# Fused attention, soft mixture of experts and feed-forward layer: the first head's keys are loaded from ScalarE's queue, and its query pairs are added by VectorE

## Chip, core and metric

One core of a Trainium2 chip runs the whole program in one launch. The metric is the device time of one execution in microseconds (us). The kernel before took 743.18, 743.3 and 743.6 us in three timed runs; the median is 743.3.

## What is computed

Three stages follow each other. Attention has 32 heads (batch 4, 8 heads), 1152 keys of width 64, and queries that are averaged in pairs first, so 576 per head:

```python
q_pool = q.reshape(B, H, S // 2, 2, D).mean(axis=3)
scores = scale * np.matmul(q_pool, k.transpose(0, 1, 3, 2))
attn = np.exp(scores - np.max(scores, axis=-1, keepdims=True))
attn = attn / (np.sum(attn, axis=-1, keepdims=True) + 1e-09)
out = np.matmul(attn, v)
```

Then a soft mixture of experts (8 experts with 4 slots each: `logits = x @ phi`, softmax over the tokens into the slots, two weight matrices per expert, softmax over the slots back to the tokens), and last a layer `g(h) @ w_out` with `h = x @ w_in` (2304 tokens, 512 to 2048 to 512) and a piecewise g. All inputs and outputs are float32.

## The kernel before

The program is written out by hand for each engine: one block each for SyncE, GpSimd, TensorE, ScalarE and VectorE, each a list of instructions in fixed order. Engines meet only through semaphores (`wait_ge` on one side, `then_inc` on the other); a finished DMA adds 16.

Attention runs head by head. Per head, TensorE transposes keys and summed query pairs (`turn`, L576 to L598; `turn(m, 0)` holds the first eight key tiles at L585, `turn(m, 1)` the queries at L590 and the tail tiles at L594 and L596), multiplies for the row maxima (`row_max`, L600), turns the negated maxima (L634), multiplies scores (`scores`, L657 to L663), weighs the values (L680) and adds up the sums (L691). ScalarE rounds the transposed keys and queries to the high part (`high`, L1086; `round_k`, `round_q`) and takes the exponentials (L1072). VectorE computes the low part as a difference (`low`, L1328) and the row maxima (L1356). GpSimd adds the two queries of each pair (`prepare`, L469 to L476) and adds up exponentials. While head n is in its scores, head n+1 is in its maxima and head n+2 is being loaded.

Three buffers matter here. `k_raw` and `q_raw` take the keys and queries of one head as loaded, each by two DMAs: a large one (288 KB for keys, 256 KB for queries) and a small one of 32 KB. `q_pool` takes the added pairs. There is one of each, so head m's load waits until head m-1 has been read: a load of keys waits for `turned`, which counts two transposing jobs per head, and a load of queries for `q_pooled`. GpSimd's `prepare(m)` waits for `q_loaded` and, from head 1 on, for `turned`.

The start is a prologue of its own. SyncE issues `load_q(0)`, `load_k(0)`, `load_k(1)`, `load_q(1)` and `load_v(0)` (L371 to L375). GpSimd makes the identity `ident` (L464 to L466), waits for a small memset of VectorE (`mask_ready`) and prepares heads 0 and 1. TensorE transposes the identity 14 times into a bank that nothing reads (`warm(14, 0)`, L728), then does head 0's transposes. More such `warm` calls stand further down, between head 0's maxima (L733, L736, L744, L746). ScalarE starts with `round_k(0)` and `round_q(0)`, VectorE with memsets and small constants up to `consts_ready` (L1306 to L1325), then `low_k(0)` and `low_q(0)`, which wait for ScalarE. From L749 on the loop over the heads runs.

The end of the kernel has the only DMA that ScalarE issues (L1300): half of the last output tile, while SyncE issues the other half (L457).

Of the kernel before, what the change touches and what calls it, by code (L numbers as in the profile page):

```python
# [8 lines left out]
ALU = mybir.AluOpType  # L9
# [7 lines left out]
def soft_moe_chain(nc, q, k, v, phi, w1, w2, w_in, w_out, out):  # L17
# [13 lines left out]
    B, H, S, D = k.shape  # L31
# [3 lines left out]
    NT = S // P  # L35
    QT = 5
# [3 lines left out]
    PAIRS = H // 2  # L40
    TOK = B * SQ
    E, _, FE = w1.shape
    SLOTS = phi.shape[1]
    SPE = SLOTS // E
# [15 lines left out]
    def at(name, shape, offset, dt=F32):  # L60
        return nc.alloc_sbuf_tensor_at(name, shape, dt, offset=BASE + offset)


    QF = QT - 1
# [20 lines left out]
    k_raw = at("k_raw", [P, NT + 1, D], AFT)  # L85
    q_raw = at("q_raw", [P, QT, 2 * D], AFT + 2560)
    q_pool = at("q_pool", [P, QT + 1, D], AFT + 5120)
# [81 lines left out]
    with ExitStack() as ctx:  # L169
        ps = ctx.enter_context(nc.psum_tensor("ps", [P, 8, BANK], F32))  # L170

        def sem(name):
            return ctx.enter_context(nc.semaphore(name))

        ident_ready = sem("ident_ready")
        mask_ready, consts_ready = sem("mask_ready"), sem("consts_ready")
        k_loaded, q_loaded = sem("k_loaded"), sem("q_loaded")
        v_loaded = [sem(f"v_loaded{i}") for i in range(2)]
        q_pooled, rounded = sem("q_pooled"), sem("rounded")
        turned, turn_free = sem("turned"), sem("turn_free")  # L180
# [55 lines left out]
        k_dram = k.rearrange("b h (p j) d -> (b h) p j d", p=P)  # L236
# [99 lines left out]
        @block.sync  # L336
        def _(sp):
            def load_k(m):
                if m > 0:
                    sp.wait_ge(turned, 2 * m)  # L340
                sp.dma_start(k_raw[:, 0:NT, :], k_dram[m]).then_inc(k_loaded, 16)
                sp.dma_start(k_raw[:, NT, :], k_dram[m][:, NT - 1, :]).then_inc(k_loaded, 16)

            def load_q(m):
                if m > 0:
                    sp.wait_ge(q_pooled, m)
                sp.dma_start(q_raw[:, 0:QT - 1, :], q_big[m]).then_inc(q_loaded, 16)
                sp.dma_start(q_raw[0:QLAST, QT - 1, :], q_small[m]).then_inc(q_loaded, 16)
# [20 lines left out]
                                 inv_dram[:, HALF * h:HALF * h + HALF].to_broadcast([D, HALF])).then_inc(inverses_back, 16)  # L369

            load_q(0)  # L371
            load_k(0)
            load_k(1)
            load_q(1)
            load_v(0)  # L375
# [12 lines left out]
            for n in range(HEADS):  # L388
                if n + 2 < HEADS:
                    load_q(n + 2)  # L390
                    load_k(n + 2)
                if n + 1 < HEADS:
                    load_v(n + 1)
                if n == HEADS - 1:
                    sp.wait_ge(turned, 2 * HEADS)
                    sp.wait_ge(q_pooled, HEADS)
                    load_piece(PRE + STAGED)
                    sp.wait_ge(scores_ready, NT * (HEADS - 1))
                    for i in range(STAGED_EARLY):
                        load_piece(PRE + i)  # L400
                if n > 0:
                    turn_sums(n - 1)
                if 4 <= n < 4 + PRE:
                    load_piece(piece_first_in(n - 4))
# [58 lines left out]
        def _(pool):  # L463
# [5 lines left out]
            def prepare(m):  # L469

                pool.wait_ge(q_loaded, 32 * m + 32)
                if m > 0:
                    pool.wait_ge(turned, 2 * m)
                nc.gpsimd.tensor_tensor(q_pool[:, 0:QT, :], q_raw[:, :, 0:D], q_raw[:, :, D:2 * D], ALU.add)
                nc.gpsimd.tensor_tensor(q_pool[:, QT, :], q_raw[:, QF, 0:D], q_raw[:, QF, D:2 * D],
                                        ALU.add).then_inc(q_pooled, 1)  # L476
# [13 lines left out]
            def head(n):  # L490
                sums = (p_sum[:, :], p_sum2[:, :])
                if n > 1:
                    pool.wait_ge(q_pooled, min(n + 2, HEADS))
                    divide_x(n - 2)
                if n + 2 < HEADS:
                    prepare(n + 2)
                pool.wait_ge(exp_done, NT * n + 3)
                if n > 0:
                    pool.wait_ge(sums_done, n)
                    pool.wait_ge(probs_added, ADDS * n)  # L500
                nc.gpsimd.tensor_tensor(sums[0], probs[:, NT - 1, :], probs[:, 0, :], ALU.add).then_inc(probs_added, 1)  # L501
                pool.wait_ge(exp_done, NT * n + 5)
                nc.gpsimd.tensor_tensor(sums[1], probs[:, 1, :], probs[:, 2, :], ALU.add).then_inc(probs_added, 1)
                if n == HEADS - 1:
                    pool.wait_ge(probs_added, ADDS * n + 1)
                    nc.gpsimd.tensor_tensor(sums[0], sums[0], probs[:, 3, :], ALU.add).then_inc(probs_added, 1)
                else:
                    for u in (3, 4, 5):
                        pool.wait_ge(exp_done, NT * n + 5 + u // 4 * 2)
                        pool.wait_ge(probs_added, ADDS * n + u - 2)  # L510
                        total = sums[(u + 1) % 2]
                        nc.gpsimd.tensor_tensor(total, total, probs[:, u, :], ALU.add).then_inc(probs_added, 1)  # L512
                last = ADDS if n < HEADS - 1 else LAST_ADDS
                pool.wait_ge(probs_added, ADDS * n + last - 1)
                nc.gpsimd.tensor_tensor(sums[0], sums[0], sums[1], ALU.add).then_inc(probs_added, 1)

            pool.wait_ge(mask_ready, 1)
            prepare(0)
            pool.wait_ge(q_pooled, 1)
            nc.gpsimd.memset(q_neg[1][:, :].bitcast(F32), 0.0).then_inc(zeroed, 1)  # L520
            pool.wait_ge(zeroed, 1)
            prepare(1)
            for n in range(HEADS):
                head(n)
# [531 lines left out]
        def _(act):  # L1056
# [28 lines left out]
            def high(dst, src):  # L1085
                nc.scalar.activation(dst, src, ACT.Copy).then_inc(rounded, 1)  # L1086

            def round_k(m):
                act.wait_ge(turned, 2 * m + 1)
                high(k_hi[m % 2][:, 0:KP], ps[:, 6, :])  # L1090

            def round_q(m):
                kh, qh, b = k_hi[m % 2], q_hi[m % 2], tail_bank(m)
                act.wait_ge(turned, 2 * m + 2)
                for g in range(2):
                    for odd in range(2):
                        high(by_turns(qh, g, odd), turned_q(odd))
                high(kh[:, KP:KP + P], ps[:, b, 0:P])
                high(qh[:, P * QF:SQ], ps[:, b, P:P + QLAST])

            def place_neg_max(m):
# [4 lines left out]
                                                scale=neg_mask[0:r, t:t + 1])  # L1106
                last.then_inc(neg_free, 1)

            round_k(0)
            round_q(0)  # L1110
            round_k(1)
# [192 lines left out]
        def _(dve):  # L1304
# [18 lines left out]
                                  sum_ident[:, :].unsqueeze(1).to_broadcast([P, P // SLOTS, SLOTS]))  # L1323
            nc.vector.tensor_tensor(neg_mask[:, :], ident[:, 0:QT], ident[:, D:D + QT], ALU.add).then_inc(consts_ready, 1)
            dve.wait_ge(consts_ready, 1)  # L1325

            def low(dst, src, hi):
                return nc.vector.tensor_tensor(dst, src, hi.bitcast(F32), ALU.subtract)  # L1328
# [304 lines left out]
```

## Time and profile before

| | |
|---|---|
| timed runs, us | 743.18, 743.3, 743.6 |
| span of the profiled execution (first to last instruction), us | 738.7 |
| time of the profiled execution outside its span | not listed by itself; the timed runs lie 4.5 to 4.9 us above this span |
| TensorE busy | 724.9 us, 98% |
| VectorE, ScalarE, GpSimd busy | 71%, 62%, 66% |
| TensorE's share of the chain that ended last | 93% |
| mean granted TensorE clock | 0.995 of full |

The busy time is an average over all stages. The chain that ended last is followed back from the last instruction to what released it; a piece of it that gets shorter makes the kernel shorter until another wait ends later. In the names, PE is TensorE's matmuls, PEld its weight loads, DVE VectorE, ACT ScalarE, POOL GpSimd, SPq and ACTq the queues of SyncE and ScalarE where DMAs are issued. L12 is line 12 of the kernel.

### The profile page before, as it was taken

What the parts mean: (1) busy time and instruction counts of PE and PEld (TensorE: products, weight loads), DVE (VectorE), ACT (ScalarE), POOL (GpSimd) and SP (SyncE); (2) the same over time, 40 slices, a digit from 0 to 9 for tenths busy, and PEclk for the clock granted to TensorE, in tenths of its full rate; (3) what the DMA queues carried; (4) which work ended last, traced back from release to release, by engine and by line L of the source; (5) the groups of instructions that cost most, each with busy time, mean ns of one, the idle gap of its engine ahead of it and who ended that gap; (6) DMA issues with size and microseconds to landing.
All of it is one profiled execution on the core that took longest, in us unless ns stands there. A gap on an engine that the chain in (4) does not pass through costs nothing.

```text
span 738.7 us, 17096 instructions
## 1 busy us (share of the span) xinstructions
PE 724.9 (98%) x6375; PEld 540.5 (73%) x6375; DVE 523.4 (71%) x826; ACT 455.6 (62%) x1008; POOL 485.1 (66%) x431
## 2 busy tenths in 40 slices
PE   7999999999999999999999999999999999999997
PEld 5776777777777777777777677434778888888886
DVE  6888888888888888888888847533894555455542
ACT  3677776776777767767767763214655454545453
POOL 2588888888888888888888873212774444444442
PEclk8999999999999999999999999999999999999999
DMA  5123335334244353353342347899301010101011
GB/s 142 47 59 100 106 95 157 99 111 151 88 120 143 91 155 105 98 164 88 112 151 88 96 140 259 298 387 387 132 1 43 1 43 0 43 0 43 0 43 43
DMA packets 51623, 81.83 MB, mean 111 GB/s; under 512 B 14556, under 2 KB 20572, under 8 KB 51548
## 3 DMA queue, kind: packets, MB, share of 16 engines
q1 hardware_dynamic: 51468, 80.69, 35.0%
q8 instruction: 48, 0.79, 0.4%
q14 instruction: 27, 0.22, 0.1%
q10 hardware_dynamic: 80, 0.13, 0.0%
HBM read 75.94 MB, written 4.79 MB: 109 GB/s over the span
## 4 chain that ended last, share of the span: by engine, by line
PE 93%; DVE 3%; ACT 1%; issue 1%; POOL 1%; DMA 0%; SPq 0%; DVEq 0%; POOLq 0%; ACTq 0%
PE ps L680 20%; PE ps L657 8%; PE ps L987 8%; PE ps L986 8%; PE ps L985 8%; PE ps L625 6%; PE ps L659 5%; PE ps L661 5%; PE ps L663 5%; PE ps L691 3%; PE ps L585 3%; PE ps L975 2%; PE ps L899 2%; PE ps L869 2%; PE ps L590 1%
## 5 line engine op out<-in xcount | busy, mean ns | idle before, releaser
L1072 ACT ACTIVATE probs<-ps 128x576 f32<-128x576 f32 x288 | 183.8, 652 | 44.0 <-PE ps L663 28.9
L1356 DVE TENSOR_REDUCE mx<-ps 128x2 f32<-128x1024 f32 (+1 forms) x160 | 189.2, 1217 | 29.1 <-PE ps L625 27.1
L551 POOL TENSOR_TENSOR g_lo<-g_buf,g_hi 128x384 fp32r<-128x384 f32 x96 | 102.1, 1066 | 100.8 <-ACT g_hi L1245 100.8
L680 PE MATMUL ps<-probs,v_sb 128*64 128x288 f32 x1152 | 146.8, 409 | 0.1
L512 POOL TENSOR_TENSOR p_sum<-p_sum,probs 128x576 f32<-128x576 f32 x93 | 129.1, 1413 | 0.0
L1584 DVE SCALAR_TENSOR_TENSOR v_buf<-u_buf 128x384 f32<-128x384 f32 x96 | 60.2, 627 | 86.7 <-ACT u_buf L1238 86.1
L680 PEld LDWEIGHTS ps<-probs,v_sb 128*64 128x64 f32 x1152 | 79.7, 137 | 56.3 <-issue 5.2
L1238 ACT ACTIVATE u_buf<-ps,half 128x384 f32<-128x384 f32 x96 | 55.8, 582 | 93.7 <-PE ps L975 93.7
L985 PE MATMUL ps<-wo_hi,g_hi 128*128 128x512 f32 x282 | 110.5, 392 | 0.6 <-POOL g_lo L551 0.4
L987 PE MATMUL ps<-wo_lo,g_hi 128*128 128x512 f32 x282 | 110.8, 393 | 0.0
L986 PE MATMUL ps<-wo_hi,g_lo 128*128 128x512 f32 x282 | 110.6, 392 | 0.0
L657 PE MATMUL ps<-q_hi,k_hi 64*128 64x288 f32 x576 | 101.1, 335 | 0.7 <-ACT q_neg L1105 0.7
L659 PE MATMUL ps<-q_hi,k_lo 64*128 64x288 f32 x576 | 88.0, 292 | 0.0
L661 PE MATMUL ps<-q_lo,k_hi 64*128 64x288 f32 x576 | 87.9, 292 | 0.0
L663 PE MATMUL ps<-q_neg,k_one 64*128 64x288 f32 x576 | 87.3, 289 | 0.0
L501 POOL TENSOR_TENSOR p_sum<-probs 128x576 f32<-128x576 f32 x32 | 45.6, 1426 | 52.9 <-ACT probs L1072 52.9
L625 PE MATMUL ps<-k_hi,q_hi 64*128 64x512 f32 x320 | 70.6, 428 | 2.9 <-DVE mx L1356 1.6
L657 PEld LDWEIGHTS ps<-q_hi,k_hi 64*128 64x128 f32 x576 | 55.4, 184 | 23.8 <-ACT probs L1072 21.5
L985 PEld LDWEIGHTS ps<-wo_hi,g_hi 128*128 128x128 f32 x282 | 53.0, 188 | 14.3 <-issue 2.7
L1328 DVE TENSOR_TENSOR q_lo<-ps,q_hi 64x256 fp32r<-64x256 f32 (+1 forms) x160 | 60.5, 379 | 2.0 <-ACT q_hi L1086 0.7
L987 PEld LDWEIGHTS ps<-wo_lo,g_hi 128*128 128x128 f32 x282 | 52.9, 188 | 11.5
L659 PEld LDWEIGHTS ps<-q_hi,k_lo 64*128 64x128 f32 x576 | 57.3, 185 | 2.9
(214 smaller groups left out, 1251.6 us busy)
## 6 DMA issues: line engine op xcount, KB each, us to landing
pre<-in_moe_w SPq DMA_DIRECT2D x41, 512.0 KB, 4.7
k_raw<-in_k SPq DMA_DIRECT2D x32, 288.0 KB, 3.8
v_sb<-in_v SPq DMA_DIRECT2D x32, 288.0 KB, 2.8
q_raw<-in_q SPq DMA_DIRECT2D x32, 256.0 KB, 3.9
from_x<-in_moe_w SPq DMA_DIRECT2D x9, 512.0 KB, 5.2
p_inv<-inv_dram SPq DMA_DIRECT2D x62, 72.0 KB, 2.6
out<-o_stage SPq DMA_DIRECT2D x34, 128.0 KB, 2.4
staged<-in_moe_w SPq DMA_DIRECT2D x8, 512.0 KB, 5.2
```

The lines of the kernel that those rows point to most:

```text
L512: nc.gpsimd.tensor_tensor(total, total, probs[:, u, :], ALU.add).then_inc(probs_added, 1)
L625: mm = pe.matmul(ps[:, job_bank(m, j) + g, :], q_hi[m % 2][rows_of(g), P * t:P * t + P], k_hi[m % 2][rows_of(g), 0:KP], start=True, stop=True)
L657: mm = pe.matmul(out, k_hi[n % 2][rows, t], q_hi[n % 2][rows, cols], start=True, stop=False)
L659: mm = pe.matmul(out, k_lo[n % 2][rows, t], q_hi[n % 2][rows, cols], start=False, stop=False)
L661: mm = pe.matmul(out, k_hi[n % 2][rows, t], q_lo[n % 2][rows, cols], start=False, stop=False)
L663: mm = pe.matmul(out, k_one[rows, :], q_neg[n % 2][rows, cols], start=False, stop=True)
L680: mm = pe.matmul(ps[D * h:D * h + D, 4, 0:HALF], v_sb[n % 2][:, u, :], probs[:, u, HALF * h:HALF * h + HALF], start=(i == 0), stop=(i == N ...
L985: pe.matmul(o, g_hi[par][:, f, toks], wo_hi[:, f, :], start=(f == 0), stop=False)
L986: pe.matmul(o, g_lo[par][:, f, toks], wo_hi[:, f, :], start=False, stop=False)
L987: mm = pe.matmul(o, g_hi[par][:, f, toks], wo_lo[:, f, :], start=False, stop=(f == NF - 1))
L1072: nc.scalar.activation(dst, ps[:, b0:b0 + 2, 0:HALF], ACT.Exp, scale=SCORE_SCALE).then_inc(exp_done, 1)
L1356: top = nc.vector.tensor_reduce(mx[0:w, NC * t:NC * t + 2], ps[0:w, b:b + 2, :], AX.X, ALU.max)
```

## The change

The two DMAs that load head 0's keys are issued by ScalarE, as the first entries of its list after the helpers, and no longer by SyncE. Head 0's query pairs are added by VectorE, behind its constants, with the same two additions that GpSimd's `prepare(0)` made. GpSimd's wait for `mask_ready` goes; the memset that it waited for is on VectorE's own list ahead of the additions. `load_k` and `prepare` are now called for heads from 1 on only, and their waits lose the test for head 0.

```diff
         def _(sp):
             def load_k(m):
-                if m > 0:
-                    sp.wait_ge(turned, 2 * m)
+                sp.wait_ge(turned, 2 * m)
...
             load_q(0)
-            load_k(0)
             load_k(1)
...
             def prepare(m):
                 pool.wait_ge(q_loaded, 32 * m + 32)
-                if m > 0:
-                    pool.wait_ge(turned, 2 * m)
+                pool.wait_ge(turned, 2 * m)
...
-            pool.wait_ge(mask_ready, 1)
-            prepare(0)
             pool.wait_ge(q_pooled, 1)
             nc.gpsimd.memset(q_neg[1][:, :].bitcast(F32), 0.0).then_inc(zeroed, 1)
...
+            nc.scalar.dma_start(k_raw[:, 0:NT, :], k_dram[0]).then_inc(k_loaded, 16)
+            nc.scalar.dma_start(k_raw[:, NT, :], k_dram[0][:, NT - 1, :]).then_inc(k_loaded, 16)
             round_k(0)
             round_q(0)
...
             dve.wait_ge(consts_ready, 1)
+            dve.wait_ge(q_loaded, 32)
+            nc.vector.tensor_tensor(q_pool[:, 0:QT, :], q_raw[:, :, 0:D], q_raw[:, :, D:2 * D], ALU.add)
+            nc.vector.tensor_tensor(q_pool[:, QT, :], q_raw[:, QF, 0:D], q_raw[:, QF, D:2 * D],
+                                    ALU.add).then_inc(q_pooled, 1)
```

## Rows read from the trace of the kernel before

**Rows 1.** The page: busy time of each engine, and the chain that ended last by engine.

```profile
PE 724.9 (98%) x6375; PEld 540.5 (73%) x6375; DVE 523.4 (71%) x826; ACT 455.6 (62%) x1008; POOL 485.1 (66%) x431
...
PE 93%; DVE 3%; ACT 1%; issue 1%; POOL 1%; DMA 0%; SPq 0%; DVEq 0%; POOLq 0%; ACTq 0%
```

**Rows 2.** Chain of waits in order of time, 0 to 45 us: start, us, what.

```profile
2.44 2.94 DMA k_raw<-in_k
...
6.72 0.26 ACT q_hi L1086
...
19.63 0.40 PE ps L657 x2
...
28.61 4.52 PE ps L680 x36
```

**Rows 3.** Timeline, SyncE: start us, us, engine, line, operation, out<-in.

```profile
0.74 0.40 SPq L347 DMA_DIRECT2D q_raw<-in_q  x1
...
1.83 0.57 SPq L341 DMA_DIRECT2D k_raw<-in_k  x1
```

**Rows 4.** Timeline, TensorE's matmuls from 3.7 us; in brackets idle before, releaser.

```profile
3.72 1.06 PE L728 MATMUL ps<-ident 128*128 128x128 f32 x4
5.43 0.66 PE L585 MATMUL ps<-ident,k_raw 128*128 128x128 f32 x4 [0.65 <-DMA k_raw<-in_k]
```

**Rows 5.** Timeline, ScalarE, GpSimd and VectorE up to 7 us.

```profile
0.74 1.28 ACT L1086 ACT_TABLE_LOAD   x1 [0.74 <-PEq L1622]
...
3.77 0.86 POOL L474 TENSOR_TENSOR q_pool<-q_raw 128x320 f32<-128x320 f32 x1 [2.30 <-DMA q_raw<-in_q]
4.59 0.32 POOL L475 TENSOR_TENSOR q_pool<-q_raw 128x64 f32<-128x64 f32 x1
...
6.13 0.60 ACT L1086 ACTIVATE k_hi<-ps 128x512 fp32r<-128x512 f32 x1 [4.11 <-PE ps L585]
...
6.83 0.69 DVE L1328 TENSOR_TENSOR k_lo<-ps,k_hi 128x512 fp32r<-128x512 f32 x1 [3.75 <-ACT k_hi L1086]
```

**Rows 6.** Stretches: length, busy us by engine, granted clock, DMA share, GB/s.

```profile
1.75:2.75 1.00, 1.00 (x6) 1.00 (x6) 0.96 (x6) 0.27 (x1) 0.00 (x0) 1.00 0.86 236
2.75:3.75 1.00, 1.00 (x7) 1.00 (x6) 0.30 (x2) 0.00 (x0) 0.00 (x0) 1.00 0.74 131
3.75:4.75 1.00, 1.00 (x5) 0.63 (x3) 0.00 (x0) 0.00 (x0) 0.97 (x2) 1.00 0.71 244
4.75:5.40 0.65, 0.03 (x1) 0.00 (x0) 0.00 (x0) 0.00 (x0) 0.59 (x2) 1.00 0.07 19
```

**Rows 7.** DMA issues by line, 730 to 739 us: KB each, median us to landing.

```profile
out<-o_last SPq DMA_DIRECT2D x1, 128.0 KB, 2.3
out<-o_last ACTq DMA_DIRECT2D x1, 128.0 KB, 2.6
```

**Rows 8.** Lines L728 (1 to 5 us) and L585 (5 to 6.5): ns min/median/max.

```profile
L728 PE MATMUL ps<-ident x14: 421/421/477, 1.5 to 4.4; 128*128 128x128 f32 x14
...
L585 PE MATMUL ps<-ident,k_raw x4: 272/273/331, 5.4 to 5.8; 128*128 128x128 f32 x4
```

**Rows 9.** VectorE's additions and subtractions: L1388, and L1328 up to 20 us.

```profile
L1388 DVE TENSOR_TENSOR p_rest<-probs x1: 896/896/896, 443.9 to 443.9; 128x576 f32<-128x576 f32 x1
...
L1328 DVE TENSOR_TENSOR q_lo<-ps,q_hi 128x64 fp32r<-128x64 f32 x2 | 0.4, 215 | 0.0
```

**Rows 10.** Stretches around the low clock, columns as in rows 6.

```profile
12.00:12.10 0.10, 0.10 (x4) 0.10 (x1) 0.10 (x1) 0.00 (x0) 0.10 (x1) 0.77 0.08 10
12.10:18.80 6.70, 6.26 (x28) 4.22 (x25) 6.11 (x14) 3.32 (x11) 1.86 (x4) 0.50 0.60 167
18.80:18.90 0.10, 0.10 (x1) 0.00 (x0) 0.10 (x1) 0.10 (x2) 0.00 (x0) 0.60 1.02 343
```

**Rows 11.** Timeline, 15 to 18 us: two operations that waited.

```profile
15.12 0.69 DVE L1350 TENSOR_REDUCE mx<-ps 128x4 f32<-128x512 f32 x1 [0.53 <-PE ps L620]
...
17.41 0.48 PE L634 MATMUL ps<-ident,neg_max 128*128 128x128 f32 x1
```

## The prediction

> **What bounds the kernel now.** I read the page first: TensorE is busy for 98% of the 738.7 us span and is 93% of the chain that ended last [rows 1]. So a change pays only if it moves TensorE's work as a whole. The chain in order of time shows where that can happen: until about 20 us it jumps between a DMA, ScalarE, VectorE and TensorE, and from the first head's weighing at 28.61 us it is TensorE without a gap [rows 2]. The change touches only the first 7 us. An advance that survives to the first scores matmul at 19.63 us shifts all that follows by as much, because every later load, addition and exponential waits for a semaphore of this same stream of work and none for a point in time.
>
> The head of the chain is the first load of keys: SyncE issues it as its third and fourth DMA (1.83 and 2.44 us), it lands at 2.44 + 2.94 = 5.38, the transposes of L585 start at 5.43, ScalarE rounds the keys from 6.13 and the queries from 6.72 [rows 2 to 5]. TensorE's row before it says what is late next: its 14 transposes of the identity (L728) end at 4.78, and only 0.65 us idle stands before L585, released by the DMA [rows 4]. That 0.65 us, or little more, and not the 1.1 us by which the load can be issued earlier, is the size of the prize.
>
> **Part 1: the keys' two DMAs leave SyncE for ScalarE.** Removed from SyncE: two issues, the first of 0.57 us [rows 3]. Nothing there gets earlier by it: what follows there is the second head's keys, whose load waits until both transposing jobs of the first head have ended (`turned` at 2), with or without the change. Added on ScalarE: two issues ahead of everything it does. Its engine is free: one table load at 0.74 for 1.28 us, then idle for 4.11 us until 6.13 [rows 5]. Put first, they start at 0.74 and, with SyncE's durations for them, at 0.74 + 0.57 + 0.04 = 1.35, instead of 1.83 and 2.44: 1.09 us earlier. The table load then runs from about 1.8 to 3.1 and is hidden.
>
> Issued 1.09 us earlier, the keys land at 5.38 - 1.09 = 4.29 if nothing disturbs them. But now they run beside the queries, issued in the same microsecond. The DMA windows show the engines busy for 0.86 + 0.74 + 0.71 + 0.05 = 2.36 us of each engine's time between 1.75 and 5.4, with only 0.07 x 0.65 = 0.05 us of it behind 4.75, so the last bytes come near 4.85 and the semaphore at 5.38 [rows 6]. The same work at the fullest share shown for a microsecond (0.86) takes 2.74 us from 1.75, to 4.49, which is 0.36 earlier: landing at 5.02. Packed without a gap it takes 2.36, to 4.11: landing at 4.64. Bounds 4.29 and 5.38 (no gain at all); I take 4.75, nearer to the packed case, since two queues leave fewer gaps than one. The nearest row for two DMAs issued at one moment on the two queues is the end of the kernel: 128 KB each, 2.3 us to landing on SyncE's and 2.6 on ScalarE's [rows 7]; ScalarE's queue is no slower than some tenths.
>
> The Trainium skill bears on this: DMA: Bandwidth & Descriptors, section "Issuing engines are not separate DMA queues", says that DMAs started from different engines share the same 16 DMA engines and interleave, and that using several saves only the sequencer's time to issue them. By that rule the gain is at most the 1.09 us of issue, no time below 742.2 comes out, and the queries' bytes take their part of it; the trace before can't show it for loads, since all of them go through one queue.
>
> **What is late next.** TensorE's warm-up. Its last four matmuls take 1.06 us, the last alone 0.42, so they follow each other by (1.06 - 0.42) / 3 = 0.21; the last starts at 4.36 and ends at 4.78, and the next can start near 4.6 [rows 4, 8]. With the keys at 4.75 + 0.05 the first transposes start at 4.8, 0.63 us earlier.
>
> Part of this is paid back by the clock. The 14 warm transposes take 421 ns each, those of L585 272 [rows 8]: the first ran at the low level (1.2 GHz) although the granted clock reads 1.00 in their rows [rows 6], the second at the high one (2.4). The rise lies between 4.4 and 5.43. Transposes started at 4.8 meet it either way. If it is there already, nothing is lost; if it comes only at 5.43, the four take 3 x 0.21 + 0.42 = 1.05 us instead of 0.66, 0.4 lost. I take 0.15, since a rise in the middle of the 0.6 us leaves one or two slow ones. Gain at the rounding of the keys: 0.63 - 0.15 = 0.48, bounds 0.2 and 0.8 (the start at 4.6).
>
> **Part 2: the query pairs are added by VectorE.** Removed from GpSimd: 0.86 + 0.32, from 3.77 to 4.91 [rows 5]. Before, this was early: the keys' transposes began 0.5 us behind it. After part 1 it would nearly bind (4.91 against the queries' first transpose at 4.8 + 0.4), so moving it protects the gain rather than adds to it. VectorE's two additions are not in the trace; its row for 128x576 in SBUF takes 896 ns and that for 128x64 215 [rows 9], so 1.33 ns a column: 0.55 us for the 128x320 one and 0.2 for the 128x64 one, 0.75 together; bounds 384 x 1.33 = 0.5 (nothing fixed per instruction) and 1.18 (GpSimd's own). With the queries landing where they did (3.7) that ends at 4.5. Delayed by the keys to 4.75 it ends at 5.5; the four transposes of queries and ends then end some 0.7 later (four of L585 take 0.66 [rows 4]), 6.2, while ScalarE, rounding the keys for 0.6 from about 5.65, wants them at 6.25. Covered by 0.05; I count nothing, and 0.15 in the bad case. Behind the waiting addition on VectorE stands only the low part of the keys, which came at 6.83 after 3.75 us of idleness [rows 5] and now comes near 6.35. Its constants are done where that idleness begins, 6.83 - 3.75 = 3.08, before the queries land. GpSimd's memset of q_neg and second preparation follow the sum's semaphore and the second load, as before. The wait that load_k and prepare lose their `if` for is no new wait for any head above 0.
>
> **Sum.** 0.5 us off the first 20. Up to 19.63 the rest is work of engines released by each other, and part of it is TensorE at the low clock (granted 0.50; the shares 0.77 and 0.60 of the slices at its ends put it from 12.05 to 18.88 [rows 10]); all of it moves along. Span 738.7 - 0.5 = 738.2. The three timed runs lie 4.5 to 4.9 above the span; with the median's 4.6 that is 742.8 us. A difference under 0.2% (1.5 us) is what a measurement of this kernel can't tell from no change, so this is "same".
>
> **Rivals.**
> 1. The clock comes back later (slower). The granted clock falls at 12.05, when TensorE has just had idle stretches, and rises at 18.88, 0.75 before the first scores [rows 10]. The first scores now come at 19.1. For: the rise leads them by 0.2 only, if it keeps its time, and nothing ties it to the work. Against: the activity before it is the same, moved by half a microsecond. Price: time at the low level does half its work, so each us of it behind 19.1 loses 0.5 where TensorE bounds. The change turns slower than before once it lasts 1.0 us beyond, and slower by 0.2% from 4.0 us beyond. Half of the whole low stretch again (3.4 us) loses 1.7: 744.0.
> 2. The clock doesn't fall, or falls later. Then L620 no longer keeps VectorE idle for 0.53 us, and L634 takes 0.27, as a transpose at the high level, instead of 0.48 [rows 8, 11]: 0.7 us more, 742.1. For: less idleness before 5.4. Against: the idle pieces behind 7 us are unchanged.
> 3. ScalarE's table load goes first, so the change doesn't do what it says. The load's row bears the line of the first activation, but ran at 0.74, long before that was released [rows 5], so its place against the DMAs is open. Then they start at 2.06 and 2.67, 0.23 later than now: 743.5. It decides once the second issue starts behind 2.44. The Trainium skill, ScalarE: Activation LUTs, section "Step-by-step: what each stage is for", says that the compiler has placed the load right before the ACTIVATE that needs it; by that, the DMAs go first and the forecast stands. No row here decides it.
> 4. The transfers are hidden in each other: both sets land where the keys did, about 5.2 to 5.4, and the additions now end near 6.0. Then VectorE's sum is late for ScalarE by some tenths: 743.3, no gain. The shares of 0.6 to 0.9 in the windows speak against that much [rows 6].
>
> **How the numbers follow.** Forecast (gain 0.2 to 0.9): 0.6. Rival 1: 0.1, of which 0.04 beyond 744.8. Rival 2: 0.1, of which 0.04 below 741.8. Rival 3: 0.1. Rival 4: 0.1. So faster by over 0.2% 0.04, slower 0.04, same 0.92. The range takes rivals 2 to 4 and the cheap half of rival 1, and the 0.4 us by which the three runs differ: 741.9 to 743.7.
>
> **What would show it.** Two DMA issues on ScalarE at 0.74 and 1.35, the table load behind them; L585 starting near 4.8, perhaps with matmuls of 421 ns among its four; VectorE's sum of 0.75 us ending by 5.5; the first scores near 19.1; the same distance from there to the end. Wrong if L585 stays at 5.4, if ScalarE's first issue is at 2.06, if the clock's rise stands behind the first scores, or if the time leaves 741.8 to 744.8.

## The result, and the profile after

In 22 timed runs each, taken in turns on one chip, the kernel before has a median of 743.21 us (740.4 to 744.57) and the changed one 741.5 us (739.76 to 742.72): ratio 0.9981, 95% interval 0.9973 to 0.9989, so 0.8 to 2.0 us faster. Two more comparisons gave 0.9988 (0.9976 to 1.0) and 0.9984 (0.997 to 0.9997). The three together put the gain at 0.9 to 1.4 us; the second interval just reaches no gain. Forecast were 0.5 us and 742.8, with a range from 741.9; the time lies below it. All runs that count here are of one state; one single run of the kernel before, beside the later experiments, took 2024.64 us and is in no median or ratio.

Each run now comes with its span. Over 46 runs of the changed kernel the time is 1.8 us above the span, and it is 1.8 us for before too (the prediction used 4.6). So the profiled execution of before, with its span of 738.7, took about 740.5 us by that distance: it was as quick as the fastest of the 22 runs (740.4), and not one like the median. The changed kernel's profiled execution took 741.45 us with a span of 739.7. Set side by side, the two profiles show the change as 1.0 us slower. That is the first thing to know before comparing their lines.

The page of the changed kernel, busy time and chain that ended last (answers to [rows 1]):

```profile
PE 726.1 (98%) x6375; PEld 541.8 (73%) x6375; DVE 524.3 (71%) x828; ACT 455.1 (62%) x1008; POOL 483.7 (65%) x429
...
PE 94%; DVE 3%; issue 1%; POOL 1%; ACT 1%; POOLq 0%; DVEq 0%; ACTq 0%
```

Its timeline up to 7 us (answers to [rows 3 to 5]; L580 is L585 of before, L585 is L590, L1081 is L1086):

```profile
0.74 0.41 ACTq L1104 DMA_DIRECT2D k_raw<-in_k  x1
...
1.19 0.46 ACTq L1105 DMA_DIRECT2D k_raw<-in_k  x1
...
1.67 1.28 ACT L1081 ACT_TABLE_LOAD   x1 [1.67 <-PEq L1623]
...
4.57 1.11 PE L580 MATMUL ps<-ident,k_raw 128*128 128x128 f32 x4
4.76 0.49 DVE L1324 TENSOR_TENSOR q_pool<-q_raw 128x320 f32<-128x320 f32 x1 [1.68 <-DMA q_raw<-in_q]
5.17 0.22 DVE L1325 TENSOR_TENSOR q_pool<-q_raw 128x64 f32<-128x64 f32 x1
5.44 0.29 PEld L585 LDWEIGHTS ps<-ident,q_pool 128*128 128x128 f32 x2 [0.17 <-DVE q_pool L1325]
...
6.60 1.59 ACT L1081 ACTIVATE q_hi<-ps 64x256 fp32r<-64x256 f32 x4 [0.28 <-PE ps L591]
```

The keys are issued first and the table load runs behind them. The keys land at 1.19 + 3.3 = 4.5, and in this profile the warm-up (which ends at 4.78, as before) is what the transposes follow. The queries are no longer there at 3.77 but at 4.76, and VectorE's sum ends at 5.39, when TensorE has waited 0.17 us for it. ScalarE rounds the queries at 6.60, against 6.62 in the timeline of before (6.72 in its chain [rows 2]): next to nothing was won in this profile up to there, because the four transposes took 1.11 us and not 0.66 [rows 4] and those of the queries behind them were slow too.

The granted clock of the changed kernel (answers to [rows 10], columns as in rows 6):

```profile
16.00:17.00 1.00, 0.53 (x4) 0.29 (x3) 0.97 (x5) 0.00 (x0) 0.56 (x2) 0.92 0.86 299
17.00:23.00 6.00, 5.33 (x36) 4.82 (x37) 4.75 (x10) 2.68 (x7) 0.00 (x0) 0.50 0.26 77
23.00:24.00 1.00, 1.00 (x13) 0.93 (x11) 0.84 (x2) 0.65 (x1) 0.19 (x1) 0.66 0.00 0
...
474.00:480.00 6.00, 6.00 (x46) 1.71 (x42) 0.32 (x2) 0.00 (x0) 0.00 (x0) 0.72 1.05 403
```

The low stretch is as long as in the first profile, 6.8 us, but lies from 16.84 to 23.68 and so inside the first head's scores (which start at 18.95, not 19.63). A second one lies at the start of the experts' first product (0.72 on average from 474 to 480), which takes 15.4 us instead of 13.8. Rivals 1 and 2 of the prediction are about such stretches. They turn up in the profiles of both kernels below, so an experiment has to hold them still before the change can be measured. (The product's time here and below is from the start of its first matmul to that of its last.)

### The profile page after: what moved, and what is told of

Read it like the earlier page. It is cut to its first block, busy times and chain, and to the rows that moved or that the text cites. A ratio compares the mean times of both kernels' runs of the same rounds, so it can differ in the third digit from the quotient of the medians.

```text
span 739.7 us, 17095 instructions
## 1 busy us (share of the span) xinstructions
PE 726.1 (98%) x6375; PEld 541.8 (73%) x6375; DVE 524.3 (71%) x828; ACT 455.1 (62%) x1008; POOL 483.7 (65%) x429
## 4 chain that ended last, share of the span: by engine, by line
PE 94%; DVE 3%; issue 1%; POOL 1%; ACT 1%; POOLq 0%; DVEq 0%; ACTq 0%
PE ps L675 20%; PE ps L652 9%; PE ps L982 8%; PE ps L981 8%; PE ps L980 8%; PE ps L620 6%; PE ps L654 5%; PE ps L656 5%; PE ps L658 5%; PE ps L686 3%; PE ps L580 3%; PE ps L970 2%; PE ps L864 2%; PE ps L894 2%; PE ps L585 1%
## 5 line engine op out<-in xcount | busy, mean ns | idle before, releaser
L982 PEld LDWEIGHTS ps<-wo_lo,g_hi 128*128 128x128 f32 x282 | 53.0, 188 | 11.4
```

What stands on the lines that cost most here:

```text
L982: mm = pe.matmul(o, g_hi[par][:, f, toks], wo_lo[:, f, :], start=False, stop=(f == NF - 1))
```

## The experiments

Two theories follow from these profiles: **prologue** (the order of loads and sums is shorter by itself) and **clock** (the change moves low-clock stretches). Times are medians; ratios are to the kernel before on the same chip.

### The two kernels again

> The kernel before, unchanged, against itself. The profile that the prediction used had a span of 738.7 us at a mean granted clock of 0.995, while 22 runs have a median of 743.2; the changed kernel's runs lie 1.75 us above their spans. Clock theory: the spans of typical runs are near 741.4 us at a mean clock under 0.990, and the new profile shows more low-clock time in the first 30 us than the 6.8 us of the first one. Prologue theory (the time was won in the order of loads and sums, the clock is the same for both kernels): clocks like the changed kernel's, 0.988 to 0.995. Ratio 1.000 within 0.001 by both.

Measured: 742.55 us, ratio 0.9995 (0.9986 to 1.0004); mean clocks of single runs 0.988 to 0.999. Its profile is another one than that of [rows 2 to 5]. The chain of waits:

```profile
2.44 2.84 DMA k_raw<-in_k
...
5.33 1.11 PE ps L585 x4
6.44 0.43 PE ps L590 x2
...
7.33 0.38 ACT q_hi L1086
```

The keys land as before, but TensorE stays at its low level through all of their and the queries' transposes, and the queries are rounded at 7.33, 0.7 later. The low stretch goes from 14.1 to 24.3. Span 740.8, which is what the median less 1.8 gives; the first profile was 2 us below that. The clocks of single runs are not all under 0.990, as the clock theory had them.

> The kernel before again: ratio 1.000 within 0.001. The first weighing near 30 us, not the 28.5 of the first profile, if that one was a lucky case; the experts' product either 13.8 or 15.4.

Measured: 742.94, ratio 0.9997 (0.9981 to 1.0012). Queries rounded at 7.44, low from 12.5 to 26.1, first weighing at 31.3 (later than the expected 30), experts 15.4, span 742.4. Of three profiles of this kernel the first is the quickest, a lucky case.

> The changed kernel again, on one chip with the three below. In the first profile of before the queries landed at 3.7 us and the keys' transposes ran at the high clock; in a second profile of the same kernel they landed at 4.5 and the transposes took 1.11 instead of 0.66 us, so the first was a good case. Prologue theory: at equal granted clock the changed kernel is 0.3 to 0.6 us shorter, because late queries no longer meet GpSimd's 1.14 us sum and a late start of the keys; ratio 0.9992, time 0.6 below before. Clock theory: the spread of 4 us between runs is where the low-clock stretch falls, and more than 1 us of the 1.7 us is a better mix of it: ratio 0.998, and a mean clock of the runs clearly above that of before.

Measured: 741.89, ratio 0.9988 (0.9976 to 1.0). Queries rounded at 6.53, weighing at 29.2, experts 13.8, span 738.9. Its runs' clocks (mostly 0.988 and 0.993) are no better than before's: the mean over all 46 runs of the changed kernel is 0.991, over 136 of before 0.993. In every trace the record of the granted clock begins only where the level first rises. The low start ahead of it is read as 1.00, so the mean clock doesn't order the kernels: in the 136 runs of before, those at 0.998 have spans from 738.2 to 742.8.

> The changed kernel again. Own-gain theory with two clocks: 0.8 to 1.4 us below before, the first weighing near 29.2 us in the profile, the experts' product either 13.8 or 15.4.

Measured: 742.11, ratio 0.9984 (0.997 to 0.9997). Queries rounded at 6.38, weighing at 30.2 (the forecast of 29.2 missed: low from 11.4 to 25.1), experts 15.4.

### Each half alone

> Head 0's keys from ScalarE's queue, the pairs still added by GpSimd. Both theories: keys land near 4.5, queries near 4.7, GpSimd's sum of 1.14 us ends at 5.9, so ScalarE's rounding of the queries starts at 7.1, 0.5 later than in either kernel. Clock theory: the idle 0.65 us in front of the keys' transposes is gone, so most of the 1.7 us stays: 741.8 to 742.3. Prologue theory: 0.5 us slower than before, 743.7.

Measured: 741.87, ratio 0.9998 (0.9987 to 1.0009). Before took 742.18 beside it. Queries rounded at 7.52, later than expected; the time is inside the clock theory's range, but the ratio shows no gain and no loss: neither theory's size came. Its profile shows why a mean clock misleads: it reads 0.998, and yet TensorE's first rise comes only at 20.46 us. And the end of this kernel is 0.4 us shorter than before (see the table below), which hides part of what the late queries cost.

> Head 0's pairs added by VectorE, the keys still on SyncE's queue. Keys land at 5.38 as before, TensorE idles 0.65 us before their transposes, the sum ends near 4.5 and is not waited for. Clock theory: same as before, 743.2 (742.8 to 743.6). Prologue theory: also 743.2, since the sum was not late. A gain of more than 0.8 us would speak against both.

Measured: 742.57, ratio 1.0001 (0.9992 to 1.001), the same as before, as both theories had it.

> The kernel before with 17 instead of 14 identity transposes at the start, so that TensorE is busy until about 5.4, when the keys land; no load or sum is moved. Clock theory (what TensorE's idle 0.65 us at 4.8 did to the granted clock later is what the change removed): 741.5 to 742.2, mean clock like the changed kernel's. Prologue theory: 743.2, or 0.1 to 0.2 us more where the keys' transposes wait for the last of the 17.

```diff
-            warm(14, 0)
+            warm(17, 0)
```

Measured: 742.25, ratio 1.0002 (0.9993 to 1.0011). The clock theory in this form falls: filling the idle 0.65 us alone gives nothing by the ratio, with a low stretch from 11.5 to 25.2 all the same. The interval leaves room for 0.5 us, so a small gain of this edit isn't excluded.

### The keys hold up the queries

> The changed kernel with ScalarE issuing the keys' DMAs only when the queries have landed. If the keys' packets are what delays the queries (4.7 us in the changed kernel's profile), the queries land by 3.4 to 3.8 here and the keys 2.5 to 3 us later, 6.2 to 6.8, and TensorE idles for them. If the queries' landing varies by itself, it may be anywhere from 3.4 to 4.7. Time 1 us longer or more: 742.5 to 744.

```diff
+            act.wait_ge(q_loaded, 32)
             nc.scalar.dma_start(k_raw[:, 0:NT, :], k_dram[0]).then_inc(k_loaded, 16)
```

Measured once: 745.37 us, above the expected 742.5 to 744; a single run says little of the time. Its timeline does say something:

```profile
3.83 0.49 DVE L1325 TENSOR_TENSOR q_pool<-q_raw 128x320 f32<-128x320 f32 x1 [0.75 <-DMA q_raw<-in_q]
...
6.85 1.12 PE L580 MATMUL ps<-ident,k_raw 128*128 128x128 f32 x4 [2.08 <-DMA k_raw<-in_k]
```

Queries at 3.8 here; at 4.76 to 5.20 in all six profiles of the changed order and at 5.06 to 5.18 with the keys alone on ScalarE's queue; at 3.7 to 4.6 where SyncE issues all four. So keys that are issued beside the queries make these land later: the means over the profiles of the changed order and of those in which SyncE issues all four are 5.0 and 4.0, 1.0 us apart. The Trainium skill's page DMA: Bandwidth & Descriptors, section "Issuing engines are not separate DMA queues", says that DMAs started from different engines interleave on the same 16 DMA engines, and the traces of the changed order agree: in each of its six profiles both sets land within 0.3 us of each other.

### The clock held up

More identity transposes go where TensorE waits for ScalarE or VectorE, in both kernels ("more": the first three lines; "full": all).

```diff
             turn(0, 1)
-            warm(5, 0)
+            warm(12, 0)
             row_max(0, 0)
             row_max(0, 1)
-            warm(5, 0)
+            warm(12, 0)
...
-            warm(5, 5)
+            warm(8, 5)
...
             slot_sums_of_tails()
+            warm(7, 1)
             pe.wait_ge(fold_w_ready, 1)
...
+            warm(3, 1)
             pe.wait_ge(sim_ready, 1)
```

> The changed kernel with more identity transposes in TensorE's gaps of the prologue: 12, 12 and 8 in place of 5, 5 and 5. They fit into waits for VectorE or ScalarE at the high clock (0.11 us each). Clock theory: the low stretch between 11 and 25 us goes or gets shorter, the spread between runs shrinks, and the time is 1 to 2 us below the changed kernel's (739.8 to 740.5). Prologue theory alone: no gain, or up to 0.5 us slower where a transpose at the low level (0.21 us) delays the maxima.

Measured: 739.46, ratio 0.9961 (0.9947 to 0.9975), runs from 739.28 to 740.18. The stretches of its profile:

```profile
5.00:12.00 7.00, 5.83 (x40) 4.57 (x41) 4.90 (x9) 2.50 (x7) 1.24 (x2) 1.00 0.52 140
12.00:19.00 7.00, 4.66 (x34) 3.06 (x33) 6.92 (x15) 3.88 (x12) 1.68 (x4) 1.00 0.60 173
19.00:26.00 7.00, 6.73 (x79) 5.71 (x79) 6.39 (x9) 4.32 (x7) 2.73 (x2) 1.00 0.01 2
```

No low stretch is left up to 26 us; TensorE is busy 5.8 us from 5 to 12, and 4.4 in the first profile of the changed kernel. The time is 2.4 us below the changed kernel on the same chip; the same fill takes 2.4 and 2.0 us off the kernel before (743.07 to 740.64, 742.54 to 740.58). So the low stretches cost both kernels 2 to 2.4 us.

> The kernel before with the same additional identity transposes. If they hold the clock up in both, the difference between this and the changed kernel with them is the change's own gain without the clock. Prologue theory: 0.3 to 0.6 us slower than the changed kernel with them. Clock theory (the change works through the clock): no more than 0.2 us apart.

Measured: 740.64, ratio 0.9971 (0.9959 to 0.9984): 1.2 us above the changed kernel with the same transposes. That is more than the prologue theory had and far from the clock theory's 0.2: the change has a gain that doesn't hang on the later low stretches.

> The changed kernel with 12, 12 and 8 identity transposes in TensorE's gaps, again, now on one chip with both halves of the change alone and with neither, all with the same transposes. Interaction theory (with the clock held up, the change is worth about 1 us, and only both parts together are): 739.5, and 1.0 to 1.3 us below the kernel before with them. Rival (one part alone does it): one of the two halves reaches this time.

> The kernel before with the same identity transposes, again. Interaction theory: 740.6. Rival: the same.

> Only the keys on ScalarE's queue, GpSimd adds the pairs, with the same identity transposes. Interaction theory: the queries land near 5.1 behind the keys, GpSimd's sum of 1.14 us ends near 6.3, ScalarE rounds the queries no earlier than in the kernel before (7.4 to 7.5): 740.4 to 740.8. Rival (the earlier keys do it alone): 739.5 to 739.8.

> Only the pairs on VectorE, the keys on SyncE's queue, with the same identity transposes. Interaction theory: the sum wasn't waited for, since the keys' transposes start near 5.4: 740.4 to 740.8. Rival (the faster sum does it alone): 739.5 to 739.8.

Measured on one chip: both parts 739.14 (ratio 0.9958, 0.9943 to 0.9973), neither 740.58 (0.9975, 0.9965 to 0.9985), keys alone 740.21 (0.9969, 0.9956 to 0.9982), pairs alone 740.67 (0.998, 0.9969 to 0.9991). Only both together do it; the keys alone may do a third (their mean over 6 runs is 740.19, standard error 0.24, against 740.58, 0.12, over 19 runs of neither on two chips), which is as much as their shorter end gives (table below). What holds the keys back when alone is the old sum:

```profile
5.06 0.86 POOL L472 TENSOR_TENSOR q_pool<-q_raw 128x320 f32<-128x320 f32 x1 [3.58 <-DMA q_raw<-in_q]
...
5.88 0.32 POOL L473 TENSOR_TENSOR q_pool<-q_raw 128x64 f32<-128x64 f32 x1
...
6.25 0.69 PE L588 MATMUL ps<-ident,q_pool 128*128 128x128 f32 x2 [0.35 <-POOL q_pool L473]
```

Queries at 5.06, GpSimd's sum until 6.2, TensorE idle for it: the queries are rounded at 7.40, as where the rise is late in before.

> The changed kernel with the identity transposes in the prologue and 7 and 3 more in TensorE's two gaps (0.79 and 0.38 us) before the experts' first product. Gap theory (the granted clock falls at the experts because of these two gaps): the product takes 13.8 us in the profile and the runs' slower cluster, 1 us above the fast one, goes: median 739.0 to 739.3. Rival (the fall comes from the narrow matmuls before them): 15.4 us in some profiles still, median 739.3 to 739.5, or slower by up to 0.3 us where the transposes delay the products.

Measured: 739.22, ratio 0.9948 (0.9928 to 0.9968), the lowest ratio of all, 3.9 us below before (743.07). The ten transposes before the experts bring at most some tenths of it: without them 739.46 and 739.14 were measured in other comparisons. With TensorE's gaps before the experts filled, their product takes 13.8 or 13.9 us in all four profiles that have this; without, 15.3 to 15.5 in 11 of 16.

```profile
470.00:474.00 4.00, 3.98 (x36) 2.21 (x34) 1.82 (x8) 0.00 (x0) 0.63 (x1) 1.00 1.05 400
474.00:480.00 6.00, 6.00 (x58) 2.00 (x62) 0.32 (x2) 0.00 (x0) 0.00 (x0) 1.00 1.04 398
```

> The kernel before with all the same identity transposes. Own-gain theory: 0.5 to 0.7 us slower than the changed kernel with them, because the prologue is later by that (keys half a microsecond, and slow transposes in front of the queries' rounding), and the rest of the 1.0 us seen between the two before was the experts' clock. Rival (all of the 1.0 us is the prologue): 0.9 to 1.2 us slower.

Measured: 740.62, ratio 0.9966 (0.9954 to 0.9978): 1.4 us above, more than either expectation. The timelines of the two, first this one, then the changed one:

```profile
5.44 1.11 PE L585 MATMUL ps<-ident,k_raw 128*128 128x128 f32 x4 [0.67 <-DMA k_raw<-in_k]
...
7.45 0.78 ACT L1088 ACTIVATE q_hi<-ps 64x256 fp32r<-64x256 f32 x2 [0.26 <-PE ps L596]
```

```profile
4.79 0.66 PE L580 MATMUL ps<-ident,k_raw 128*128 128x128 f32 x4
...
6.38 0.78 ACT L1083 ACTIVATE q_hi<-ps 64x256 fp32r<-64x256 f32 x2 [0.29 <-PE ps L591]
```

1.07 us apart here, 1.1 at the first scores (19.71 and 18.61) and 1.07 at the first weighing (28.74 and 27.67). In the one TensorE is still at its low level, in the other it has risen. From 7 to 10 us its identity transposes, in this kernel and in the changed one:

```profile
L728 PE MATMUL ps<-ident x12: 421/421/422, 7.2 to 9.5; 128*128 128x128 f32 x12
```

```profile
L723 PE MATMUL ps<-ident x18: 272/273/328, 6.8 to 9.9; 128*128 128x128 f32 x18
```

The clock's record begins at 10.29 here and at 4.47 there. The added transposes hold up the first maxima here (they start at 9.90, without idle time before them, and at 9.08 in the profile of before_third, which rises late too), but that costs nothing: VectorE works on low parts until 10.80 in both and takes its first maximum then.

> The kernel before with all the identity transposes except those three, on the same chip: 740.5 by both theories, the queries' rounding at 7.4 in the profile in two cases of three.

> The kernel before with all the identity transposes of before_full_warm and 17 instead of 14 at the start, so that TensorE isn't idle before the keys land. Gap theory (the 0.65 us idle stretch holds the clock down over the first transposes; the change removed it): the keys' transposes start at 5.3 to 5.5 and the queries are rounded by 6.7 in the profile, and the time is 0.5 us or more below before_full_warm: 739.6 to 740.0. Rival (the rise comes when it comes): no difference, 740.4 to 740.7.

Measured on one chip: 739.62 (0.9964, 0.995 to 0.9977) without the three transposes more at the start, and 739.74 (0.9965, 0.9953 to 0.9977) with them. The same kernel that took 740.62 took 739.62 in its five runs here, with the queries rounded at 6.60. Its 17 spans lie in two groups: seven from 737.7 to 738.3 (mean 737.9) and ten from 738.8 to 739.1 (mean 738.9). The two profiles of this kernel fit that: the one with the early rise (5.23) has a span of 737.9, the one with the late rise 738.8. All five runs of this comparison are in the quick group. So there was no late rise for the three added transposes to remove, to judge by the spans, and the run doesn't decide.

### Four numbers from all 20 profiles

| order | queries rounded at, us | four key transposes, us | TensorE's first rise, where the clock's record begins, us (in the order of the second column) | last activation's start to the span's end, us |
|---|---|---|---|---|
| keys on SyncE's queue, idle stretch before the keys (9; two of them with the pairs on VectorE) | 6.35, 6.45, 6.53, 6.60, 6.62; 7.33, 7.44, 7.45, 7.45 | 0.66 in the first five; 1.11 or 1.12 in the others | 4.58, 4.56, 4.71, 5.23, 5.23; 7.25, 9.07, 9.42, 10.29 | 4.05 to 4.09 |
| the same, idle stretch filled (2) | 6.50, 6.75 | 0.66, 0.89 | 4.71, 5.85 | 4.08, 4.08 |
| keys on ScalarE's queue, pairs on VectorE (6) | 6.38, 6.38, 6.41, 6.53, 6.60, 6.75 | 0.66 in three, 1.11 or 1.12 in three | 4.47 to 4.87 in the first three; 5.98, 6.61, 6.28 | 3.68 to 3.70 |
| keys alone on ScalarE's queue (2) | 7.40, 7.52 | 1.11, 1.12 | 10.85, 20.46 | 3.69, 3.70 |

The kernel in which the keys wait for the queries is the twentieth (8.86; 1.12; 10.32; 3.69).

The last column is a gain that no step of the prediction has. In full warm-up, before and after:

```profile
734.72 0.60 ACT o_last L1300
```

```profile
733.25 0.60 ACT o_last L1297
```

with spans of 738.80 and 736.93: from there 4.08 and 3.68 us. It is 0.4 us in every profile with the keys on ScalarE's queue, and in none with the pairs alone moved. The last two DMAs themselves are alike (2.3 and 2.6 us to landing, as in [rows 7]), and the time is saved behind them, on SyncE. When its wait for the output has ended, SyncE has a branch and then a drain, behind which all engines meet and the span ends. From the start of the branch to that of the drain the trace has 0.46 us in all eleven profiles with the keys on SyncE's queue and 0.15 in all nine others, and the drain takes 0.08 and 0.01 us. That is 0.38 together. ScalarE's own drain has ended more than 1.5 us before that in both.

## Why the prediction was wrong

**The level: wrong, without harm to the sum.** "The three timed runs lie 4.5 to 4.9 above the span" joined runs to a profile of another, faster execution; the runs show 1.8. The sum stayed near the right level only because a change of 0.5 was put on the median. What was missed by it is that the profiled execution was 2.8 us from the median, more than the whole effect, and that its prologue could not be taken as the usual one. The rows on record then could not show this; a second profile would have.

**What is late next: right in the start, not in what binds.** L580 starts at 4.57 to 4.99 (forecast 4.8), but the chain of waits up to the queries' rounding runs through the warm-up in only one of the six profiles of the changed order. In two it runs through the keys' landing, in three through the queries' landing and VectorE's sum. GpSimd's sum would be late, as foreseen: with the keys alone moved the queries are rounded at 7.40 and 7.52.

**Landing.** Keys forecast at 4.75, measured 4.5 to 4.95. Queries: taken for landing "where they did (3.7)", with 4.75 as the bad case; it is the only case (4.76 to 5.20). VectorE's sum took 0.63 (forecast 0.75); TensorE waits for it by 0.2 us in four of the six profiles and not at all in the two others. The bound of 1.09 us from the earlier issue held for the keys (landed at 5.1 to 5.4 before); the time fell below 742.2 by what follows.

**"Gain at the rounding of the keys: 0.63 - 0.15 = 0.48": this step failed, though its number is near.** It counts a load that comes earlier, in a profile of before in which TensorE has risen when the keys are transposed. Against that case the keys are rounded 0.42 earlier in the changed kernel's first profile (5.71 and 6.13), but the queries are not: the mean of the five is 6.51, that of the six too. The first weighing is no earlier either. With no low stretch behind the start it comes at 27.64 and 27.82 in the two profiles of the old order that rise by 4.71, and at 27.67, 27.71 and 28.05 in the three of the changed order. The gain that is there stands against the case that the prediction didn't know: in four of nine profiles TensorE rises only at 7.25 to 10.29, and the queries are rounded at 7.4, 0.9 later (7.42 - 6.51). In all six of the changed order it has risen by 6.61. Over the nine this makes 0.4. That the sum's 0.5 is close to it is luck.

**A missing term: 0.4 us at the kernel's end**, in every profile. The prediction put the rest of the kernel at nothing ("the same distance from there to the end"); the distance from the last activation to the end fell from 4.08 to 3.69.

0.4 + 0.4 makes 0.8 us, of the 1.0 (740.21 - 739.20, standard error 0.2) that the two kernels differ by in full warm-up, and of the 0.9 to 1.4 measured without. The 17 spans of before in full warm-up close the sum better: the seven quick ones lie 0.5 above the mean of the changed kernel (737.9 and 737.4), which is the end's 0.4 within the errors, and the ten others 1.0 higher, which over the 17 adds 0.6. So of the 1.0 about 0.4 is the end and 0.6 the late rise, and the fill holds only the later low stretches still, not the first rise. Why the first rise is late is open (below), so the 0.6 is a share of cases and not a shortened wait.

The measured 741.5 lies 1.3 below the forecast. Of that, 0.4 is the end. The rest can't be taken apart: it is within what the medians of one kernel differ by between comparisons. The prediction stood on 743.3, while other comparisons had medians of 742.2 to 743.2 for before, and 741.9 and 742.1 for the changed kernel.

**Rivals.** 3 (table load first) and 4 (both sets land where the keys did) didn't happen. The price of 1 was added up wrong: 742.8 + 1.7 is 744.5, and not 744.0. 1 and 2 were taken for cases of the change; they are a draw of each execution of either kernel: low stretches of 6.8 to 13.7 us in the prologue in all six profiles of the two kernels without fill, in four of them one more at the experts. They go with the 4 us between runs: in the filled versions the runs spread by 0.2 to 2.1 us. With them, a range of 1.8 us around one profile was too narrow for one kernel, let alone for a difference.

**Open.** Why TensorE's rise from the low level comes only at 7.25 to 10.29 us in four profiles of the order of before, and by 6.61 in all of the changed order. In all eight profiles in which TensorE idled no more than 0.25 us at a time from the warm-up to the queries' transposes it had come by 6.61; in the nine with an idle stretch of 0.4 to 0.7 us it came either by 5.23, ahead of the keys' transposes, or at 7.25 and later, and with the keys alone moved (0.35 us idle near 6) at 10.85 and 20.46. This speaks for the idle stretch as the cause, but the run that was to decide didn't, so it is not shown. Open too is what of the move shortens the end. That the time is saved in SyncE's last steps speaks for SyncE's list with two DMAs less, and not for ScalarE's queue; but in every run with the one the other was changed too, so no run tells these apart.

## What to carry to other kernels

Before a sum is built on a profile, ask where its own execution stands among the timed runs: here it was 2.8 us from the median for an effect of 1. Where TensorE's clock differs between executions, fill its waits in both versions with work that nothing reads and compare those; that separated the change (1.0 us) from the later low stretches (2 to 2.4 us), and is itself the better edit: 0.9966 and 0.9964 of the time by itself and 0.9948 together with the change, which alone gives 0.9981 to 0.9988. Read where the level first rises from the durations of like matmuls, not from the clock's column. A load that was issued earlier beside another made the other land later here, so what consumes the other had to get shorter too: neither half of this change gains by itself what both do.

## What the runs showed of the hardware

- Sets of 320 and 288 KB issued at once on two queues landed together, 3.3 to 3.9 us from issue (eight profiles), where one behind the other on one queue each took 2.4 to 3.2 (eleven profiles).
- The granted clock reads 1.00 from the start although the durations (421 ns for an identity transpose, 272 behind the rise) show the low level until the rise: the record begins with the rise, at 4.47 to 20.46 us in the 20 profiles.
- Idle stretches of 0.79 and 0.38 us in front of the experts' product go with a slow product behind them (15.4 for 13.8 us) in 11 of 16 profiles, and with the stretches filled in none of four.
- With two DMAs moved from SyncE's list to ScalarE's at the start, SyncE's steps behind its last wait take 0.38 us less, 730 us later: in all nine profiles with the move and in none of the eleven without.
